# A convolution and two feed-forward layers on one core: chunk 0 in full-width steps from the beginning, chunk 1 in halves for four steps only

## The reference

```
w = softmax(weight_gen)                       # 7 taps for each of 8 heads
x1 = sum over k of w[..., k] * x_padded[s + k]   # causal, 24 features to a head
y  = relu(x1 @ w_in1) ** 2 @ w_out1
h  = y @ w_in2
out = (h * clip(h + 3, 0, 6) / 6) @ w_out2
```

## Time and profile before

| | us |
|---|---|
| median of 3 runs | 1140.42 |
| lowest, highest | 1139.95, 1142.07 |
| the profiled execution's own time | 1141.78 |
| its span (first to last instruction) | 1140.0 |
| PE busy in the span | 1128.9 (99%) |
| DVE busy | 915.4 (80%) |
| ACT busy | 671.2 (59%) |
| GpSimd busy | 3.1 (0%) |

### The profile page before, as it was taken

How to read it: one execution, slowest core, us unless ns; L and a number is a source line. 1 busy time by engine, 2 the same in 40 slices (tenths; PEclk the granted TensorE clock), 3 DMA queues, 4 the chain that set the end, 5 groups by cost and what they waited for, 6 DMA issues and landing times.

```text
span 1140.0 us, 26860 instructions
## 1 busy us (share of the span) xinstructions
PE 1128.9 (99%) x10496; PEld 1123.2 (99%) x10496; DVE 915.4 (80%) x1029; ACT 671.2 (59%) x777; POOL 3.1 (0%) x10
## 2 busy tenths in 40 slices
PE   8999999999999999999999999999999999999998
PEld 7999999999999999999999999999999999999997
DVE  6788798796978879788797978969788796986665
ACT  5787655556455565555656555565555556565554
POOL 1000000000000000000000000000000000000000
PEclk9999999999999999999999999999999999999999
DMA  7302002011020200202002020210202002010001
GB/s 214 105 12 64 6 5 74 8 37 43 0 76 4 66 14 0 76 4 71 9 16 60 4 74 6 63 17 0 76 4 68 12 10 66 0 39 5 1 15 29
DMA packets 79451, 41.35 MB, mean 36 GB/s; under 512 B 56188, under 2 KB 72572, under 8 KB 79416
## 3 DMA queue, kind: packets, MB, share of 16 engines
q1 hardware_dynamic: 79416, 40.86, 13.6%
HBM read 29.42 MB, written 11.40 MB: 36 GB/s over the span
## 4 chain that ended last, share of the span: by engine, by line
PE 96%; ACT 2%; DVE 1%; issue 1%; POOL 0%; DVEq 0%; ACTq 0%; POOLq 0%
PE h_ps L960 45%; PE y_ps L971 30%; PE y_ps L980 20%; PE h_ps L939 1%; ACT hid L442 1%; ACT hid L447 1%; PE y_ps L949 0%; ACT win L430 0%; ACT hid_hi L455 0%; DVE acc L615 0%; DVE hid_lo L737 0%; DVE hid L726 0%; DVE prod L630 0%; PE y_ps L1044 0%; DVE wout L703 0%
## 5 line engine op out<-in xcount | busy, mean ns | idle before, releaser
L960 PE MATMUL h_ps<-xt,win 64*128 64x512 f32 (+1 forms) x4860 | 1055.6, 375 | 2.2 <-DVE wout L703 1.9
L960 PEld LDWEIGHTS h_ps<-xt,win 64*128 64x128 f32 x4860 | 840.5, 185 | 2.9 <-DVE wout L703 2.1
L971 PE MATMUL y_ps<-hid_hi,wout 64*128 64x512 f32 (+1 forms) x2160 | 552.4, 375 | 2.4 <-DVE xt L711 2.4
L458 ACT ACTIVATE hid_hi<-hid 128x1024 fp32r<-128x1024 f32 (+1 forms) x244 | 256.4, 1051 | 326.8 <-DVE hid L726 163.2
L737 DVE TENSOR_TENSOR hid_lo<-hid,hid_hi 128x1024 fp32r<-128x1024 f32 (+1 forms) x270 | 313.2, 1160 | 149.1 <-ACT hid_hi L458 137.1
L971 PEld LDWEIGHTS y_ps<-hid_hi,wout 64*128 64x128 f32 x2160 | 387.3, 185 | 3.3 <-DVE xt L711 2.7
L971 PE MATMUL y_ps<-hid_lo,wout 64*128 64x512 f32 (+1 forms) x1080 | 318.2, 374 | 0.2 <-DVE hid_lo L737 0.2
L980 PE MATMUL y_ps<-hid_lo,wout 64*128 64x512 f32 (+1 forms) x1080 | 317.8, 374 | 0.0
L980 PE MATMUL y_ps<-hid_hi,wout 64*128 64x512 f32 (+1 forms) x1080 | 317.7, 374 | 0.0
L971 PEld LDWEIGHTS y_ps<-hid_lo,wout 64*128 64x128 f32 x1080 | 195.7, 185 | 0.8 <-DVE hid_lo L737 0.6
L980 PEld LDWEIGHTS y_ps<-hid_hi,wout 64*128 64x128 f32 x1080 | 195.5, 185 | 0.2
(11 more groups left out here) (92 smaller groups left out, 335.4 us busy)
## 6 DMA issues: line engine op xcount, KB each, us to landing
xwin<-in_x_dram SPq DMA_DIRECT2D x14, 960.0 KB, 5.7
by_feature<-stage SPq DMA_DIRECT2D x52, 96.0 KB, 2.0
out_dram<-outs SPq DMA_DIRECT2D x240, 16.0 KB, 1.5
out_dram<-outs SPq DMA_DIRECT2D x240, 8.0 KB, 1.4
stage<-by_feature SPq DMA_DIRECT2D x13, 256.0 KB, 3.0
stage<-in_moe_w_out_dram SPq DMA_DIRECT2D x8, 384.0 KB, 4.3
stage<-in_moe_w_in_dram SPq DMA_DIRECT2D x8, 256.0 KB, 4.0
stage<-in_moe_w_in_dram SPq DMA_DIRECT2D x16, 128.0 KB, 3.6
```

The source lines that it names most:

```text
L458: act.activation(hi, hid[:, slot, :, 0:width], ACT.Copy).then_inc(hi_done, 1)
L960: return pe.matmul(h_ps[:, s % 2, t, 0:tokens.stop - tokens.start], win[layer][r, wn, cols], src[r, xn, tokens], start=bool(rows) and n in ...
L971: return pe.matmul(ps[:, 0, tokens], wout[layer][r, tile, w_cols], src, start=bool(rows) and s == 0 and n == 0, stop=not rows and s == STE ...
```

## The change

- **Chunk 0** goes in full-width steps at once: steps 0 to 7 (`narrow`, `early`). VectorE makes the seven products for all four rows before anything else (`tap_products`), TensorE turns them in one go (`turn_product`), and two of the product buffers lie in `hid`. The two rows' products at steps 2, 5 and 6, their turn at steps 7 and 8, and their split go. `WARM`, the number of identity matmuls at the start, goes from 10 to 15, and the identity after a turned product stands only behind the third and later ones.
- **Chunk 1** has only its first four steps in halves, steps 8 to 11 and 12 to 15 (`NARROW`), then four full-width steps 16 to 19.
- **Layer 2 of chunk 0** is steps 20 to 27 (`SECOND`).
- All that stood at a step moves to the new count: chunk 1's input is turned at steps 7 and 11, chunk 2's at step 26; `GATED`, the steps whose square VectorE makes, is 10 to 13. The pieces of weights, the taps, the exponentials and the splits of chunk 0's output are placed anew. The first rows of x come in one DMA instead of two.
- The loop over the chunks is the same but for the count.

```
-    FIRST = len(SOFTMAX) + 2 * TAPS
+    FIRST = len(SOFTMAX) + TAPS
-    HALVES = 4 * STEPS
-    ALONE = HALVES + STEPS
-    GATED = range(18, 3 * STEPS)
-    WARM = 10
+    SPLIT = STEPS // 2
+    NARROW = range(STEPS, STEPS + 2 * SPLIT)
+    SECOND = 2 * STEPS + SPLIT
+    ALONE = SECOND + STEPS
+    GATED = range(10, 14)
+    WARM = 15
...
 # SyncE
-            load_rows(0, JHALF, x_own_loaded)
+            load_rows(0, J, x_own_loaded)
...
 # ScalarE
+            for g in range(SECOND):
+                if g == 7:
+                    split_x1_hi(1, xt[0], y1_ps, 0)
+                if g == 11:
+                    split_x1_hi(1, xt[0], y2_ps, 1)
+                if g == 10:
+                    copy_y(0, STEPS, y2_ps)
+                relu(g, 0, g % 2, narrow(g))
+                if g == 2:
+                    exponentials(1)
+                if g not in GATED:
+                    square(g, g % 2, narrow(g))
...
+                hidden_hi(g, g % 2, narrow(g))
...
 # VectorE, the steps of layer 1
+                if g in (7, 11):
+                    split_x1_lo(1, xt[0], (y1_ps, y2_ps)[g // 11], g // 11)
+                if g == 10:
+                    add_y(0, y2_ps)
                 if g in GATED:
                     gate(g, 0, g % 2, HALF)
...
+                if g == 3:
+                    softmax_norm(1)
+                    taps(1, [0, 1, 2], 0)
                 if g == 4:
                     weight_lo(8)
                     weight_lo(9)
+                    taps(1, [3], 0)
+                if g == 5:
                     weight_lo(10)
+                    taps(1, [4], 0)
+                if g == 6:
+                    taps(1, [5, 6], 0)
                 if g == 7:
+                    taps(1, [0, 1], 1)
                     weight_lo(11)
                 if g == 8:
+                    taps(1, [2], 1)
+                if g in (9, 10):
+                    taps(1, [2 * g - 15, 2 * g - 14], 1)
...
+                hidden_lo(g, g % 2, narrow(g))
 # VectorE, layer 2 of chunk 0
-                if s == 0:
-                    taps(2, [5])
+                if s in (0, 2, 3, 4):
+                    taps(2, [(0, 2, 3, 4).index(s) + 3])
                 if s == 1:
-                    weight_lo(PIECES + 7)
-                if s == 2:
-                    taps(2, [6])
-                if s == 3:
-                    weight_lo(PIECES + 8)
-                    weight_lo(PIECES + 9)
-                if s in (4, 5):
-                    weight_lo(PIECES + s + 6)
+                    weight_lo(PIECES + 5)
+                    weight_lo(PIECES + 6)
+                if s in (2, 3, 4, 5):
+                    weight_lo(PIECES + s + 5)
+                if s == 5:
+                    weight_lo(PIECES + 11)
...
 # TensorE
-                if g == 15:
+                if g == STEPS - 1:
                     pe.wait_ge(prep_done, prep_value(1, f"add{TAPS - 1}", 0))
                     turn_att(1, y1_ps, 0)
-                if g == 23:
+                if g == STEPS + SPLIT - 1:
                     pe.wait_ge(prep_done, prep_value(1, f"add{TAPS - 1}", 1))
                     pe.wait_ge(y_added, 1)
                     turn_att(1, y2_ps, 1)
```

More of the change, by code:

```diff
@@ L452, in hidden_hi @@
                 hi = hid_hi[:, slot, :, 0:width] if own is None else last_hi[own]
-                if isinstance(g, int) and g < HALVES and g not in GATED:
+                if isinstance(g, int) and g < SECOND and g not in GATED:
                     act.wait_ge(squared, squared_value(g))
@@ new lines, in _ @@
+            for n in range(3):
+                split_piece(n)
+            split_x1_hi(0, xt[1], y1_ps)
+            for n in range(3, 5):
+                split_piece(n)
+            for g in range(SECOND):
[10 more added lines that the diff above has]
+                    square(g, g % 2, narrow(g))
+                if g == 13:
+                    split_x2_main_hi(0, xt[1])
+                if g == 14:
+                    split_x2_rest_hi(0, xt[1])
+                hidden_hi(g, g % 2, narrow(g))
+                if g == 0:
+                    split_piece(6)
+                if g in (2, 3, 4, 5):
+                    split_piece(g + 6)
+                if g == 15:
+                    exponentials(2)
+                if g in (16, 17):
+                    split_piece(PIECES + 2 * g - 32)
+                    split_piece(PIECES + 2 * g - 31)
+                if g == 18:
+                    split_piece(PIECES + 4)
@@ L619, in taps @@
                         dve.wait_ge(prep_done, prep_value(c, "norm"))
-                        dve.wait_ge(att_turned, 2 if half is not None else c + 2 if isinstance(c, int) else VECTOR + 2)
+                        dve.wait_ge(att_turned, 1 if half is not None else c + 1 if isinstance(c, int) else VECTOR + 1)
                         if isinstance(c, int) and c == 1:
@@ L706, in split_x1_lo @@
             def split_x1_lo(c, dst, ps, half=None):
-                before = 2 * c + 4 if half is None else 4 * c + 2 * half
+                before = 2 * (c + (half or 0) + (c >= 2))
                 dve.wait_ge(x1_hi, before + 2)
@@ L858, in _ @@
-                if g == 18:
-                    add_y(0, y2_ps)
+                    softmax_norm(2)
+                    taps(2, [0])
+                if g == 17:
+                    weight_lo(PIECES)
+                    weight_lo(PIECES + 1)
+                if g == 18:
+                    weight_lo(PIECES + 2)
+                    weight_lo(PIECES + 3)
+                    taps(2, [1])
+                if g == 19:
+                    weight_lo(PIECES + 4)
+                    taps(2, [2])
@@ L930, in first_sums @@
                 pe.wait_ge(piece_lo, IN_PART[0])
-                for n, tile in enumerate(tiles):
-                    pe.matmul(sums(n), win[0][:, 2, tile], src[:, 2, 0:HALF], start=False, stop=False)
-                    ins = pe.matmul(sums(n), win[0][:, 3, tile], src[:, 2, 0:HALF], start=False, stop=True)
-                    if n % PAIR == PAIR - 1:
-                        ins.then_inc(mm1_done, 1)
+                for n in range(PAIR):
+                    part(n, 2, 2)
+                    ins = part(n, 3, 2, stop=True)
+                ins.then_inc(mm1_done, 1)
+                for n in range(PAIR, 2 * PAIR):
+                    part(n, 1, 0)
+                    part(n, 0, 1)
+                    part(n, 2, 2)
+                    ins = part(n, 3, 2, stop=True)
+                ins.then_inc(mm1_done, 1)
             def identities(count):
@@ L971, in main_part @@
                 return pe.matmul(ps[:, 0, tokens], wout[layer][r, tile, w_cols], src,
-                                 start=bool(rows) and s == 0 and n == 0, stop=not rows and s == STEPS - 1 and n == 5,
+                                 start=bool(rows) and s == 0 and n == 0 and half != 1, stop=not rows and s == STEPS - 1 and n == 5,
                                  tile_position=(r.start, 0))
@@ L980, in rest_part @@
                 return pe.matmul(ps[:, 1, tokens], wout[layer][r, PAIR * s + t, HI_LO_REST], src,
-                                 start=bool(rows) and s == 0 and n == 0, stop=not rows and s == STEPS - 1 and n == 3,
+                                 start=bool(rows) and s == 0 and n == 0 and half != 1, stop=not rows and s == STEPS - 1 and n == 3,
                                  tile_position=(r.start, 0))
@@ L1115, in _ @@
             for m in range(TAPS):
-                turn_product(0, m)
-                identities(1)
+                turn_product(m)
+                if m >= 2:
+                    identities(1)
             identities(3)
@@ L1149, in _ @@
                     pe.wait_ge(piece_lo, layer * PIECES + IN_PART[s // 2])
-                inn = (layer, s, xt[int(layer == 0 and g >= 2 * STEPS) ^ 1], half)
-                first_body(g, inn, late, g >= HALVES + 2)
-                if g == HALVES + LAG:
+                inn = (layer, s, xt[int(STEPS <= g < SECOND) ^ 1], half)
+                first_body(g, inn, late, g >= SECOND + 2)
+                if g == SECOND + LAG:
                     pe.wait_ge(y_added, 1)
```

233 lines of the change are left out of this document (84 added, 149 removed).

## The result

| | before | changed |
|---|---|---|
| median, us | 1141.18 (1139.95 to 1142.07, 4 runs) | 1148.51 (1147.57 to 1148.95, 4 runs) |
| the profiled execution's own time | 1141.78 | 1147.57 |
| its span | 1140.0 | 1145.8 |

The runs of before are one more than those shown ahead of the prediction. The change makes the kernel slower: 1148.51 against 1141.18 us, a ratio of 1.0064 with a 95% interval of 1.0046 to 1.0081. The two profiled executions lie 5.8 apart, the medians 7.3. The executions of the kernel before fall into two groups, near 1140.2 and near 1142.0, so its median moves by up to 2 us with the draw; the changed kernel's median is 6.4 above the slowest of these four.

The account below looks back on a forecast made before the run. TensorE, busy 99% of the span, was taken as the bound. Changes up to three marks, -9.4 +5.5 +5.9 = +2.0, with 3.85 for the clock made +5.9 us: median 1146.3, range 1138.5 to 1150.5.

Parts of the forecast that it names:

- The three turns: Input turns at steps 7, 11 and 26: TensorE waits 2.85, 4.75 and 2.3 us for VectorE's last tap sums.
- the stretch from step 7 to step 19: First to second mark, 48.8 to 92.4: new waits at steps 8, 11 and 12 give back 5.5 of 9.4 us won.
- clock term: Half-clock falls behind the waits at steps 7, 11 and 26 add 1.85, 1.35 and 0.65, together 3.85 us.
- stretches at 0.50 right behind them: Sign expected in the profile: granted clock at half right behind the turn waits of steps 7, 11 and 26.
- The start: Up to step 0's relu: products begin at 5.45, relu at 17.5 instead of 14.77, 2.7 us lost.
- The sum for the turns: Turned products at the start: three of 0.5, then four of 1.06 with identities between, the last ending at 13.6.
- Piece 10: Low part of a weight piece made late by step 2's exponentials: TensorE waits 0.75 us at step 6.
- -1.36: Offset from the profiled execution's time to the median, in us, taking 1147.7 to 1146.3.
- Rival 2: Faster: VectorE's taps are done when TensorE reaches the turns, new waits under about 8 us; 1136.5, chance 0.15.
- The rival that VectorE's work is too much in layer 2: Layer 2: VectorE does not catch up, another turn costs 2 to 4 us with a further fall; 1150, chance 0.14.
- the rule from the Trainium skill: Warm matmul cost rule: widening 12 step pairs wins 0.6 us instead of 3.2, making the sum +8.5; forecast rejected it.
- third mark: Relu of the last step of chunk 0's layer 2, step 27: forecast at 130.85, 2.0 us later than before.

Follow-up runs that it names:

- e5: Changed kernel plus unused identity matmuls keeping TensorE busy before the turns of steps 7, 11 and 26 (12, 21, 9); 1146.02 us.
- e1: Changed kernel with chunk 1's first-half taps 3 to 6 one step earlier, ahead of step 5's low part; 1145.42 us.
- e4: Changed kernel with the edits of e1, e2 and e3 together, so taps come earlier for the turns of steps 7, 11 and 26; 1139.62 us.
- e6: e4 with the split of chunk 1's turned input ahead of the high and low parts of steps 6 and 10; 1136.54 us.
- e8: e6 and e7 together, plus chunk 1's softmax and first-half taps 0, 1, 3 a step earlier and chunk 0's output copies sooner; 1132.50 us.
- e10: e8 with 10 instead of 15 warming identity matmuls at the start (`WARM`); 1132.23 us.
- e7: e4 with layer 2's list reordered: tap 5 a step earlier, weight pieces 19 to 22 done in two steps; 1136.52 us.
- e2: Changed kernel with chunk 1's second-half taps spread over steps 7, 8 and 9, none behind the rest's sum; 1143.45 us.
- e3: Changed kernel with chunk 2's taps 1 to 6 each one place earlier, the last in step 23 instead of 24; 1147.45 us.

## Why the prediction was right, and where it was not

**The sign and the mechanism held.** The forecast was 1146.3 in a range of 1138.5 to 1150.5; 1148.51 was measured. The three turns wait for VectorE's sums, as named: 3.15, 4.92 and 2.42 against the 2.85, 4.75 and 2.3 of the forecast. The wait of 1.44 at step 8 was forecast as 1.4, that of 0.64 at step 12 as 1.35; TensorE came to it late, since its clock was at 0.50 until 70.50 (1.39 in e5, where it was not). e1 to e4 show that the order was the cause of the waits at the turns, e6 that of the two behind them.

**The total is as near as it is by luck: two errors of some 2.4 cancel.** One is the stretch from step 7 to step 19, the other the clock. Set e5, the run without a fall of the clock, beside the forecast without its clock term:

| us | forecast | measured |
|---|---|---|
| relu of step 0 | 17.5 | 18.10 |
| from there to step 7 | 31.3 | 31.45 (e5) |
| to step 19 | 43.6 | 45.86 (e5) |
| to step 27 | 38.45 | 37.81 (e5) |
| what the clock added | 3.85 | 1.4 |

The relus of steps 0, 7, 19 and 27 in e5:

```profile
17.33 1.03 ACT L447 ACTIVATE hid<-h_ps 128x1024 f32<-128x1024 f32 x1 [0.69 <-PE h_ps L915]
...
48.78 1.02 ACT L447 ACTIVATE hid<-h_ps 128x1024 f32<-128x1024 f32 x1
...
94.64 1.01 ACT L447 ACTIVATE hid<-h_ps 128x1024 f32<-128x1024 f32 x1
...
132.45 1.12 ACT L447 ACTIVATE hid<-h_ps,three 128x1024 f32<-128x1024 f32 x1 [0.78 <-PE h_ps L965]
```

The clock's 1.4 is what the profiled execution of the changed kernel took longer than e5 from step 0 to step 27 (116.50 against 115.12). The rows add up to 134.7 and 134.6.

- *The clock term was over-sized for this execution.* "Falls followed both times" made a rule of two cases. The clock stayed up behind 3.15 us of wait at step 7, and 1.85 did not come; the sign "stretches at 0.50 right behind them" held at two of the three turns, and not right behind: one began inside the wait, one 1.5 us after its end. The medians, though, give the clock 2.5, and the other three executions of the changed kernel have spans of 1146.3 to 1147.2 at a mean granted clock of 0.994 instead of 0.995. That would fit one more fall in each, but no trace shows it or its place.
- *The stretch from step 7 to step 19 was under-sized by 2.3.* About 1.0 of it is not TensorE's: in steps 17 to 19 ScalarE has relu, square, high part and up to two pieces of weights, 4.1 us, where a mixed step takes TensorE 3.35, so the relus run at 4.22, 4.20 and 3.90. The forecast had checked ScalarE against a step of 4.31 only. The mark is late by it, TensorE is not, and step 20's relu follows after 3.34. That also accounts for the row to step 27, which took 0.6 less than forecast although its wait for a piece was there, 1.25 in e5 against the 1.1 of the forecast. Of the other 1.3, step 8 has 0.5 (5.28 where 3.35 and 1.4 were counted) and the turn's wait 0.17; the rest was not located.
- *The start was 0.6 later than forecast.* The forecast let the products begin at 5.45 as before, but their rows now came in one transfer, and VectorE waited 0.64 and 0.22 for it. In e5, e8 and e10 step 0's relu was at 17.2 to 17.6: the landing differs from one execution to the next. The sum for the turns also has a slip: three of 0.5 and four of 1.06 behind 7.4 make 13.1, not 13.6. The last turned product ends at 14.11 in the changed kernel and at 13.33 in e5.
- *Piece 10 cost next to nothing* in the changed kernel, where 0.75 was forecast. The wait is real, but it takes one more tap in front of it: 1.32 in e1.
- *Between the profile and the median* lies the rest: the forecast scaled by -1.36, and the changed kernel's median is 0.9 above its own profiled time. The -1.36 was the draw of three executions; with the fourth it is -0.60.

Rival 2 (faster) named what would decide: new waits of less than about 8 in all. e4 has 9.35 without a fall and ends 0.1% faster, e6 6.5 and is 0.4% faster; the point was well placed. The rival that VectorE's work is too much in layer 2 lasted until e7.

**The pace.** Half-width steps take 2.28 in the changed kernel (the relus of steps 12 to 14) and full ones 4.31 (103.95 to 108.26), as before. So the 0.27 for a pair of steps, of which the rule from the Trainium skill (TensorE: Matmul & The Clock Gate, section "Wait — 56ns, not 53.3ns?") would leave a fifth, was there to be won, and for these half-height matmuls the trace after decides against the rule once more. With the waits gone it shows: e8 has the widths of the changed kernel, and its third mark is 8.5 ahead of before.

## What to carry to other kernels

- A change that gives the bound engine fewer steps also takes away time in which the other in-order engines did their side work. Order their lists anew, by when each result is needed, before judging the change: here the same instructions took 1148.5 or 1132.5 us.
- In such a list, what is ready first goes first. The split of an input that was ready stood behind a high part that still waited for TensorE's next work, and cost 1.4 us twice.
- Check each helper engine against the shortest step in which its whole list must fit, not against the longest. And when a mark is one engine's start, look at whether that engine itself was late.

## What the runs showed of the hardware

- The clock did not fall behind every wait. It fell behind idle times of 1.91 and 2.23 us of the kernel before, which are 2.19 and 2.45 from start to start, and it stayed at 1.00 behind 3.15 us in the changed kernel and 3.16 in e2. In e3, with 3.15 us of wait at the same place (41.01 to 44.16), it was 0.50 for 6.83 us from 43.51 on. So one length of wait gives either. Nor does it set the length of the fall: around the 4.92 us before the turn of step 11 it was 6.83 in the changed kernel and 3.41 in e1. The stretches of e2, of e3 and of e1:

```profile
43.84:47.25 3.41, 3.41 (x36) 2.87 (x38) 0.00 (x0) 0.78 (x1) 0.00 (x0) 1.00 0.02 8
```

```profile
43.51:50.34 6.83, 6.18 (x36) 4.97 (x38) 0.97 (x2) 1.48 (x3) 0.00 (x0) 0.50 0.07 19
```

```profile
64.07:67.48 3.41, 3.36 (x34) 3.37 (x36) 0.00 (x0) 0.62 (x2) 0.00 (x0) 0.50 0.00 0
```

- A fall need not cost half its length: in the changed kernel 2.5 us of the 6.83 lay in the wait itself, and a part of the rest was hidden by the wait at step 12, which shrank from 1.39 (e5) to 0.64. From step 7's relu to step 19's it cost 0.9 (46.80 against 45.86 in e5), and the fall of 3.41 in e1 cost as much there (46.82). The fall of the same length at step 7 of e3 cost 2.7: from step 0's relu to step 7's it took 34.09 there and 31.40 in the changed kernel.
- The mean granted clock doesn't tell the time. Of the executions of the kernel before that ran beside e1 to e4, some at 0.997 took 1140.1 us and others 1142.3, and all but one at 0.999 took 1140.1 to 1140.3.
